# Attention and two MLPs on one core: the high parts of queries and keys placed on a wait of their own, values rounded one gap earlier, and zeros multiplied in the opening pair's pauses

## The reference

```python
q_rot, k_rot = (rotate(q), rotate(k))
scores = scale * np.matmul(q_rot, k_rot.transpose(0, 1, 3, 2))
attn = np.exp(scores - np.max(scores, axis=-1, keepdims=True))
attn = attn / (np.sum(attn, axis=-1, keepdims=True) + 1e-09)
attn_out = np.matmul(attn, v)
x = attn_out.transpose(0, 2, 1, 3).reshape(B * S, H * D)
h = x @ w_in;  y = (h * (1.0 / (1.0 + np.exp(-h)))) @ w_out
h = y @ w_in2; out = np.where(h > 0.0, h, np.exp(np.minimum(h, 0.0)) - 1.0) @ w_out2
```

## Time and profile before

| | |
|---|---|
| median of 3 runs | 550.04 us (549.96 to 550.08) |
| the profiled execution's own time | 550.01 us |
| its span (first to last instruction) | 548.2 us |
| TensorE busy | 536.9 us, 98% of the span |
| ACT, POOL, DVE busy | 69%, 63%, 53% |
| TensorE's waits that are not in rows 2 | 1.3 us at the very start, 0.9 us in all where the MLP units begin |

### The profile page before, as it was taken

The page is one execution under the profiler, slowest core; times in us unless marked ns, Lnnn a source line. Parts: engine busy times, 40 slices in busy tenths (PEclk is TensorE's granted clock), DMA queues, the critical chain, the costliest instruction groups (busy, mean ns, idle before and its releaser), DMA issues.

```text
span 548.2 us, 9533 instructions
## 1 busy us (share of the span) xinstructions
PE 536.9 (98%) x3259; PEld 525.7 (96%) x3259; DVE 290.8 (53%) x603; ACT 380.6 (69%) x829; POOL 345.7 (63%) x277
## 2 busy tenths in 40 slices
PE   8799999999999999999999999999999999999997
PEld 7688889999999999999999999999999999999997
DVE  5789865744368853537663348784344530067400
ACT  3889889967668977769886668886666653356531
POOL 5988989859746656546655754445455666566662
PEclk9999999999999999999999999999999999999999
DMA  8677665576365456444444333333334444444440
GB/s 320 191 220 200 162 198 149 165 220 183 120 169 158 123 146 182 143 121 137 120 129 132 117 112 105 112 115 120 111 120 128 127 135 122 128 119 132 134 145 29
DMA packets 45790, 79.52 MB, mean 145 GB/s; under 512 B 6832, under 2 KB 14384, under 8 KB 45744
## 3 DMA queue, kind: packets, MB, share of 16 engines
q1 hardware_dynamic: 44016, 76.57, 48.0%
q10 hardware_dynamic: 1728, 2.36, 1.2%
HBM read 63.57 MB, written 2.36 MB: 120 GB/s over the span
## 4 chain that ended last, share of the span: by engine, by line
PE 90%; ACT 4%; DMA 2%; issue 1%; SPq 1%; POOL 1%; DVE 1%; ACTq 0%; POOLq 0%
PE banks L1202 72%; PE banks L1095 5%; PE banks L1072 3%; PE banks L1078 3%; PE banks L1163 3%; PE banks L1156 2%; DMA k_raw<-k 1%; ACT prob L572 1%; PE banks L1138 1%; ACT pt L592 1%; PE banks L1116 1%; POOL k_raw L400 0%; DMA k_st<-k_raw 0%; ACT v_st L561 0%; PE banks L1165 0%
## 5 line engine op out<-in xcount | busy, mean ns | idle before, releaser
L450 POOL TENSOR_TENSOR w_lo<-w_raw,w_hi 128x512 fp32r<-128x512 f32 x192 | 247.2, 1292 | 183.5 <-ACT w_hi L649 183.4
L649 ACT CAST w_hi<-w_raw 128x512 fp32r<-128x512 f32 x189 | 117.0, 622 | 31.7 <-PE banks L1202 29.4
L1202 PE MATMUL banks<-x_lo,w_hi 128*128 128x384 f32 x384 | 128.8, 336 | 0.3 <-DVE g_lo L918 0.3
L1202 PE MATMUL banks<-x_hi,w_lo 128*128 128x384 f32 x384 | 128.6, 335 | 0.0
L1202 PE MATMUL banks<-g_hi,w_lo 128*128 128x384 f32 x384 | 128.5, 335 | 0.0
L1202 PE MATMUL banks<-x_hi,w_hi 128*128 128x384 f32 x384 | 128.5, 335 | 0.0
L1202 PE MATMUL banks<-g_lo,w_hi 128*128 128x384 f32 x384 | 128.5, 335 | 0.0
L1202 PE MATMUL banks<-g_hi,w_hi 128*128 128x384 f32 x384 | 128.5, 335 | 0.0
L787 DVE TENSOR_REDUCE neg_max<-banks 128x1 f32<-128x576 f32 x72 | 54.1, 753 | 52.7 <-PE banks L1078 51.4
L661 ACT ACTIVATE act_buf<-banks 128x384 f32<-128x384 f32 x96 | 47.4, 493 | 37.5 <-PE banks L1202 37.0
L1202 PEld LDWEIGHTS banks<-x_lo,w_hi 128*128 128x128 f32 x384 | 72.1, 188 | 1.3 <-issue 1.0
(11 more groups left out here) (119 smaller groups left out, 729.5 us busy)
## 6 DMA issues: line engine op xcount, KB each, us to landing
w_raw<-w SPq DMA_DIRECT2D x192, 256.0 KB, 2.7
q_raw<-q SPq DMA_DIRECT2D x11, 384.0 KB, 3.6
q_one<-q_raw SPq DMA_DIRECT2D x44, 96.0 KB, 2.9
k_raw<-k SPq DMA_DIRECT2D x7, 576.0 KB, 5.5
k_st<-k_raw SPq DMA_DIRECT2D x28, 144.0 KB, 2.9
v_raw<-v SPq DMA_DIRECT2D x8, 320.0 KB, 3.4
out<-act_buf ACTq DMA_DIRECT2D x12, 192.0 KB, 2.5
k_both<-k_st SPq DMA_DIRECT2D x15, 144.0 KB, 3.1
```

The costliest lines, as they stand in the source:

```text
L450: nc.gpsimd.tensor_tensor(w_st[LO][:, slot, :], w_raw[:, slot, :], w_st[HI][:, slot, :].bitcast(F32), ALU.subtract).then_inc(w_lo_done, 1)
L649: nc.scalar.copy(w_st[HI][:, slot, :], w_raw[:, slot, :]).then_inc(w_hi_done, 1)
L1202: last = nc.tensor.matmul(dst, w_st[wp][:, slot, m * P:(m + 1) * P], src[xp][:, tile, :], start=start and n == 0, stop=stop and n == 2)
```

## The change

It does three things. (1) `place_q_one` waits for `q_hi_done` in place of `q_lo_done`; `place_keys` is cut into `place_keys_hi`, which waits for `k_hi_done`, and `place_keys_lo`, which waits for `k_lo_done`; `place` calls q_one, keys_hi, q_two, keys_lo. (2) `values_hi(0)` goes from tile 2 to tile 1, between `probs_hi(0)` and `keys_hi(1)`. (3) TensorE multiplies 7 products of zeros after score tile 1, 4 after the ends of tile 1 and 2 after the end of tile 2, into banks that are overwritten later.

```diff
@@ place_q_one
-                sp.wait_ge(q_lo_done, r)
+                sp.wait_ge(q_hi_done, r)
                 sp.wait_ge(scored, QN * (i - 1))
@@ place_keys
-            def place_keys(r, par):
-                i, ready = 2 * r + par, k_placed[par]
-                rows, others = rows_of[par], other_rows_of[par]
+            def place_keys_hi(r, par):
+                i, rows = 2 * r + par, rows_of[par]
+                sp.wait_ge(k_hi_done, r)
+                sp.wait_ge(scored, QN * (i - 1))
+                sp.dma_start(k_st[rows, i % SLOTS, :].bitcast(F32), k_raw[r % 2][rows, 1, :]).then_inc(k_placed[par], 16)
+
+            def place_keys_lo(r, par):
+                i, rows, others = 2 * r + par, rows_of[par], other_rows_of[par]
                 sp.wait_ge(k_lo_done, r)
                 sp.wait_ge(scored, QN * (i - 1))
-                sp.dma_start(k_st[rows, i % SLOTS, :].bitcast(F32), k_raw[r % 2][rows, 1, :]).then_inc(ready, 16)
-                sp.dma_start(k_st[others, i % SLOTS, :].bitcast(F32), k_raw[r % 2][rows, 0, :]).then_inc(ready, 16)
+                sp.dma_start(k_st[others, i % SLOTS, :].bitcast(F32), k_raw[r % 2][rows, 0, :]).then_inc(k_placed[par], 16)
+
+            def place_keys(r, par):
+                place_keys_hi(r, par)
+                place_keys_lo(r, par)
@@ place
                 place_q_one(r, par)
+                place_keys_hi(r, par)
                 place_q_two(r, par)
-                place_keys(r, par)
+                place_keys_lo(r, par)
@@ ScalarE's loop over the first 24 tiles
                 if t == 0 and i:
                     end_hi(i - 1)
+                if n == 1:
+                    values_hi(0)
                 if i % 2 == 0:
                     if t == 0:
                         queries_hi(p + 1)
                     if t == 1:
                         keys_hi(p + 1)
-                    if t == 2:
+                    if t == 2 and i:
                         values_hi(p)
@@ TensorE
-            def zeros(count):
+            def zeros(count, dst=mlp(0)):
                 for m in range(count):
-                    nc.tensor.matmul(mlp(0), g[LO][:, FT - 1, 0:P], g[LO][:, FT - 1, :], start=m == 0,
+                    nc.tensor.matmul(dst, g[LO][:, FT - 1, 0:P], g[LO][:, FT - 1, :], start=m == 0,
                                      stop=m == count - 1)
@@
             score_tile(1)
+            zeros(7, banks[:, 4, 0:CT])
             for n in range(H * QN):
@@
                 if t >= 1:
                     transpose_end(n)
+                if n in (1, 2):
+                    zeros(6 - 2 * n, pv_out)
```

## The result

The changed kernel takes 551.17 us (median of 18 executions, 549.69 to 554.1) against 550.02 us (18 executions, 549.31 to 550.83) for the kernel before. So the change makes the kernel slower by 0.3%, where I forecast 549.6 us with 550.3 as the upper end. Those four have a mean granted clock of 0.996 or 0.997 where the others have 0.999 or 1.000, so part of their excess may not be the change's. Without them the median is 551.12 us, so this isn't what makes the kernel slower. The profiled one took 552.26 us, with a span of 550.5 us, and lies in the upper part.

A forecast was written before the change was run, and what follows sets the result against it. TensorE was taken as bound by multiplication, with only a few us of opening waits to win. Rounding (0.63 us) and placing (1.13 us) overlap to 0.41 us: 550.04 less 0.41, about 549.6 us, range 548.9 to 550.3.

The forecast's parts named there:

- The opening: Tiles 0 to 6: earlier rounding of values (0.63 us) and placing (1.13 us) overlap to 0.41 us won at transpose 7.
- the next bound: Before transposes 5: VectorE's order, with maximum 5 at 21.1 us, holds them, not the placing DMA; win there 0.47 us.
- The clock: Rival: TensorE at 1.2 GHz in the opening's pauses, so zeros win over 1 us; 548.5 us or less, 3 in 100.
- the values that hold up keys: Rival: values_hi(0) on ACT waits for its load and delays keys_hi(1); 551.2 us, 4 in 100 with other zeros mishaps.
- the whole placing coming through: Rival: VectorE not in the way, so all 1.13 us of pair 1's earlier placing arrives; 548.9 us, 12 in 100.
- Zeros ... I cost both at nothing: Opening pauses on TensorE: seven zeros (1.21 us) and four (0.69 us) are covered by awaited exponentials; cost 0, no gain.
- TensorE waited once only for a placing, in pair 1. So nothing.: Later pairs' placing: keys' low part stays last in both orders and sets the landing; no effect, 0 us.
- a time won by 27.73 is thus handed on whole: Behind transpose 7: the chain repeats every 12.91 us, so the opening's win passes undiminished into the MLP stages.
- A DMA is late: Rival: an SP issue stall falls on pair 1's placing and nothing is won; 550.0 to 550.2 us, 14 in 100.

The follow-up runs named there:

- the last version: Against the kernel before: values moved, new placing for pair 1 only, no zeros; run again on another chip, 549.3 us beside 550.01, ratio 0.999.

## Why the prediction was wrong, point by point

**The opening: right.** 0.41 us were forecast at transpose 7 and 0.41 found. The single steps, less the 0.38 us of the start: `values_hi(0)` didn't wait for its load; L293's first issue 18.3 forecast by that measure, 18.39 found; landing 2.3 us later; maximum 5 20.72 forecast, 20.73 found; transposes 5 22.4, found 22.41. The DMA was indeed not the next bound; VectorE's order was. The opening's part, without zeros and with the later pairs as before, gives 549.28 and 549.3 us.

**The clock, the values that hold up keys, the whole placing coming through:** none happened. In the profiled execution the granted clock is unchanged, and the zeros gain nothing at all.

**"Zeros ... I cost both at nothing": the step that failed.** The term was put at 0 and measured 1.1 us alone (ratio 1.0019) and, by the medians, 1.8 us in the changed kernel (551.17 against 549.36 us without them). The cover for their time on TensorE holds, as shown above. But I priced only their time. That they also shift the fetches of TensorE's code is what the traces support: with 13 products more, one fetch went from 61.58 us to between 57.3 and 58.6 in six traces, into the placing of pair 4, and 0.37 to 0.93 us were lost at score tile 24 in five of them; in the sixth nothing was. It isn't a full account. In the profiled execution of the changed kernel this fetch stayed at 61.45, and its largest loss, 1.84 us at tile 12, belongs to the next step.

**"TensorE waited once only for a placing, in pair 1. So nothing.": the second step.** I assumed that the keys' low part lands as long after its issue as before. In the new order that of pair 2 took 3.3 to 5.6 us instead of 2.4 to 3.2, and where a fetch met `q_two` as well, up to 1.84 us were lost at score tile 12. And I read the lack of a wait as slack. The keys of pair 4 landed at 60.58 us and score tile 24 began at 60.71 in the kernel before. A score tile that waits for its keys begins 0.13 or 0.14 us behind the landing (35.76 and 35.90, 61.92 and 62.06 in the changed kernel), so there was no slack at all. The waits don't show what is just in time; the landing beside the consumer's start does. The same holds for "a time won by 27.73 is thus handed on whole": it is where the placings keep their length (the keys of pair 4 landed at 59.90 in the last version, and nothing was lost), and it was lost where one of them took longer.

**The rival "A DMA is late" had the mechanism and not the size.** It took the issue of 1.71 us as something that could fall elsewhere, but only within pair 1, where it has room, and ended at 550.2 us. It was left without a cause, so I couldn't see that what causes it comes 26 times; and without the step behind it. A delay at tile 24 puts `x_lo` behind GpSimd's start, and that costs up to 2.5 us on VectorE, of which 0.15 to 1.1 us reached TensorE in five traces.

**What stays open.** The changed kernel has one trace, so how often it loses at tile 12, and how its 1.1 us divide between the zeros and the new order, isn't known. The new placing of pairs 2 to 4 cost time in the trace of it alone, but by the times it isn't told apart from nothing (0.9993 against 0.9989 without zeros, 1.0009 [1.0, 1.0018] alone). Nor is it known why the fetch moves by 1.7 us between executions of one program, as 60.39 against 58.64, why a placing with a block inside it took 2.6 us once and 3.1 to 3.3 in five other traces, and why 26 more instructions shift the fetch by up to 4 us.

## What to carry to other kernels

Work that fills a pause is free only in the engine's time; its instructions are fetched too, by DMAs that the placings meet. Where a consumer starts 0.13 us behind the landing of its DMA, any longer DMA loses what was won, so look for landings without slack before calling a stage unaffected. When the order or the start of DMAs changes, ask what loads they now run beside. A change worth 0.4 us should be measured part by part: here one part, the zeros, brought nothing and cost more than the others won. And a long GpSimd instruction with operands in SBUF is best kept away from, or cut beside, VectorE's subtractions of two SBUF operands, since a small delay can put one behind the other for its whole length.

## What the runs showed of the hardware

- A fetch of TensorE's code is one packet of 16 KB, of 0.9 to 2.4 us, every 20 us or so. A placing of pair 4's keys with one inside it took 3.1 to 3.3 us instead of 2.4 in five traces and 2.6 in one; one of 96 KB took 3.5 to 4.0 instead of 2.1 to 2.4. An issue on SP took 1.0 to 2.5 us instead of 0.3 to 0.6: all 90 issues of over 1 us in 18 traces overlap a fetch. By the Trainium skill (same page and section as above) such a refill is mostly hidden; for TensorE that held here (no pause at 24.04 in the kernel before), but not for the other queues' transfers.
- Added products of zeros didn't cost by their number: 7 alone 0, 6 alone 0, 13 alone 1.1 us.
- VectorE's subtraction of two SBUF operands took 0.54 us or, beside GpSimd's 1152-column product, 2.15 to 3.04 us, by when it starts: it got through where it began up to 0.32 us behind GpSimd's recorded start (11 traces) and waited where it began 0.42 to 0.95 us behind (5 traces). Beside half a product it took 1.0 and 1.35.
- An SBUF-to-SBUF placing of 144 KB took 2.3 to 2.4 us with little else on its way and up to 5.6 us beside loads of 960 KB.
